# Two pairs' first-half block of scores in the other half of the array's columns, with a second copy of v's first 64 rows

## The reference

```python
# B, H, S, D = 2, 8, 768, 48: r, k, v, w are [B, H, S, D], u is [H, D]
for t in range(S):
    cur = u * k[t] (outer) v[t]
    y[t] = r[t] . (state + cur)
    state = w[t] * state + k[t] (outer) v[t]
x = y as [1536, 384]
x = elu(x @ w_in) @ w_out                        # 384 -> 2048 -> 384
out = sum_e p[:, e] * (relu(x @ w1[e]) @ w2[e])  # 4 experts, 384 -> 1024 -> 384
```

## Time and profile before

| | |
|---|---|
| median of 3 runs | 646.93 us (646.88 to 647.08) |
| the profiled execution | 646.69 us, its span 644.9 us |
| PE busy | 638.4 us of the span (99%) |
| DVE busy | 418.6 us (65%) |
| ACT busy | 237.1 us (37%) |
| POOL busy | 296.0 us (46%) |

### The profile page before, as it was taken

How to read it: one execution, slowest core, us unless ns; L and a number is a source line. 1 busy time by engine, 2 the same in 40 slices (tenths; PEclk the granted TensorE clock), 3 DMA queues, 4 the chain that set the end, 5 groups by cost and what they waited for, 6 DMA issues and landing times.

```text
span 644.9 us, 13796 instructions
## 1 busy us (share of the span) xinstructions
PE 638.4 (99%) x5046; PEld 591.5 (92%) x5046; DVE 418.6 (65%) x786; ACT 237.1 (37%) x557; POOL 296.0 (46%) x370
## 2 busy tenths in 40 slices
PE   8999999999999999999999999999999999999998
PEld 5998999877788888999999999999999999999997
DVE  7889999865357666565655555565656565656564
ACT  4785555655455554222222222222222222222221
POOL 5897424420499999996029900029900018000000
PEclk9999999999999999999999999999999999999999
DMA  8954454300000233000012100013100011001011
GB/s 322 403 193 137 138 183 164 124 11 1 1 2 1 73 98 99 27 1 1 1 50 99 50 1 0 1 49 99 50 1 0 0 50 50 0 1 49 0 50 50
DMA packets 19043, 42.34 MB, mean 66 GB/s; under 512 B 2608, under 2 KB 8752, under 8 KB 18992
## 3 DMA queue, kind: packets, MB, share of 16 engines
q1 hardware_dynamic: 18704, 41.23, 18.6%
q10 hardware_dynamic: 288, 0.39, 0.2%
HBM read 37.16 MB, written 4.46 MB: 65 GB/s over the span
## 4 chain that ended last, share of the span: by engine, by line
PE 90%; DVE 4%; POOL 3%; issue 1%; DMA 0%; ACT 0%; DVEq 0%; POOLq 0%
PE bank L1365 29%; PE bank L1366 29%; PE bank L1367 29%; POOL w_lo L546 3%; PE bank L1199 1%; PE bank L1278 1%; DVE fr L863 1%; PE bank L1290 1%; DVE fr L882 1%; DVE att L921 0%; DMA rkw<-rkw_dram 0%; DVE w_lo L966 0%; DVE bank L996 0%; PE bank L1232 0%; PE bank L1298 0%
## 5 line engine op out<-in xcount | busy, mean ns | idle before, releaser
L1365 PE MATMUL bank<-x_lo,w_hi 128*128 128x256 f32 (+2 forms) x416 | 138.1, 332 | 0.5 <-POOL w_lo L546 0.3
L1366 PE MATMUL bank<-x_hi,w_lo 128*128 128x256 f32 (+2 forms) x416 | 135.2, 325 | 0.0
L1367 PE MATMUL bank<-x_hi,w_hi 128*128 128x256 f32 (+2 forms) x416 | 135.2, 325 | 0.0
L1366 PE MATMUL bank<-w_hi,g_lo 128*128 128x384 f32 x384 | 129.6, 338 | 0.0
L1367 PE MATMUL bank<-w_hi,g_hi 128*128 128x384 f32 x384 | 129.3, 337 | 0.0
L1365 PE MATMUL bank<-w_lo,g_hi 128*128 128x384 f32 x384 | 129.0, 336 | 0.0
L826 ACT ACTIVATE g_hi<-bank 128x512 fp32r<-128x512 f32 x96 | 57.5, 598 | 144.3 <-DVE bank L1052 122.4
L1365 PEld LDWEIGHTS bank<-x_lo,w_hi 128*128 128x128 f32 x416 | 78.2, 188 | 10.4 <-issue 2.5
L1367 PEld LDWEIGHTS bank<-x_hi,w_hi 128*128 128x128 f32 x416 | 78.3, 188 | 7.4
L1366 PEld LDWEIGHTS bank<-x_hi,w_lo 128*128 128x128 f32 x416 | 78.3, 188 | 7.1
L1045 DVE TENSOR_TENSOR u_sum<-p_copy,bank 128x256 f32<-128x256 f32 x56 | 23.6, 421 | 92.1 <-ACT p_copy L750 91.3
(11 more groups left out here) (134 smaller groups left out, 1258.8 us busy)
## 6 DMA issues: line engine op xcount, KB each, us to landing
raw<-w_dram SPq DMA_DIRECT2D x48, 384.0 KB, 3.7
rkw<-rkw_dram SPq DMA_DIRECT2D x10, 772.5 KB, 4.5
tok<-tok_dram SPq DMA_DIRECT2D x10, 576.0 KB, 5.9
k_blocks_dram<-k_blocks SPq DMA_DIRECT2D x8, 256.0 KB, 4.1
kt_sb<-k_blocks_dram SPq DMA_DIRECT2D x32, 64.0 KB, 2.0
out_dram<-acc SPq DMA_DIRECT2D x10, 192.0 KB, 1.9
rkw<-rkw_dram SPq DMA_DIRECT2D x2, 512.0 KB, 4.4
rkw<-rkw_dram SPq DMA_DIRECT2D x2, 260.5 KB, 3.3
```

The source lines that it names most:

```text
L1365: pe.matmul(out, wh, ml, start=start, stop=False, skip_group_check=shared)
L1366: pe.matmul(out, wl, mh, start=False, stop=False, skip_group_check=shared)
L1367: return pe.matmul(out, wh, mh, start=False, stop=stop, skip_group_check=shared)
```

## The change

For chunks 2 to 11, and in each of them for the pairs 0 and 1 (the "exchanged" pairs), the block of first-half keys by first-half queries is computed in the second half of the array's columns, so that it comes out in PSUM partitions 64 to 127, where the fully masked block lay. The fully masked block isn't computed for any pair. All blocks but one for each of the pairs 2 and 3 have now 64 queries. An exchanged pair's strips then take two matmuls of 64 queries instead of one of 128: for the first-half queries with a stationary operand whose rows 64 to 127 hold v's first 64 rows (`twice`, loaded by SP as two copies into `bonus_v_sb`), for the others with v as before. `copy_odd` copies the odd part of `twice` too. The pairs stand in another order in the score banks and in `att` (`place`), and the mask is a pair of masks, side by side; the exchanged one is put together by three more transfers. The reduction behind the diagonal writes its sums in that order.

```diff
+            def load_twice(c):
+                sp.wait_ge(s_py, c - 1)
+                sp.wait_ge(s_odd, odd_done(c - 2))
+                early = tok_d[c][0:HALF, 2 * DM:2 * DM + DM // 2]
+                sp.dma_start(twice(c), early.unsqueeze(0).broadcast_to([2, HALF, DM // 2])).then_inc(s_twice[c % 2], 16)
...
-            sp.dma_start(const[:, :], const_d).then_inc(s_const, 16)
+            sp.dma_start(const[:, P:3 * P], const_d[:, C_MASK:C_MASK + 2 * P]).then_inc(s_const, 16)
...
             load_slices(10, 11, 12, 13, 14, 15)
+            earlier, later = slice(0, HALF), slice(HALF, CH)
+            sp.dma_start(const[:, later], const_d[:, later]).then_inc(s_exchanged, 16)
+            sp.dma_start(const[earlier, earlier], const_d[later, earlier]).then_inc(s_exchanged, 16)
+            sp.dma_start(const[later, earlier], const_d[earlier, earlier]).then_inc(s_exchanged, 16)
+            load_twice(FIRST)
             sp.dma_start(probs[:, :, :], probs_d).then_inc(s_probs, 16)
             for c in range(4, NC):
                 load_rkw(c)
                 load_tok(c)
+                load_twice(c - 1)
                 move_blocks(c - 2)
+            load_twice(NC - 1)
...
+                if c >= FIRST:
+                    twice_landed(act, c)
+                    odd = twice(c).rearrange("p (a e) -> p a e", e=PD)[:, :, D:D + STRIP // 2]
+                    act.copy(v_odd[:, c % 2, PAIRS:, STRIP // 2:STRIP], odd).then_inc(s_odd, 1)
...
-                    dve.copy_predicated(att[:, o, :, :], masks.bitcast(I32), found).then_inc(s_att, 1)
+                    found = banks["x"][o][:, :].rearrange("p (a t) -> p a t", a=PAIRS // 2)
+                    dve.copy_predicated(att[:, o, :, :].rearrange("p (a b) t -> p a (b t)", b=2),
+                                        both_masks.unsqueeze(1).broadcast_to([P, PAIRS // 2, 2 * CH]).bitcast(I32),
+                                        found).then_inc(s_att, 1)
...
-                        for half in range(2):
-                            keys = slice(p * CH + HALF * half, p * CH + HALF * half + HALF)
-                            ins = pe.matmul(banks["x"][o][HALF * half:HALF * half + HALF, cols], k[rows, keys],
-                                            q[rows, cols], start=True, stop=True)
+                def block(p, o, at, keys, first, count):
+                    rows, out = slice(64 * o, 64 * o + D), place(c, p) * CH + first
+                    return pe.matmul(banks["x"][o][HALF * at:HALF * at + HALF, out:out + count],
+                                     k[rows, p * CH + HALF * keys:p * CH + HALF * keys + HALF],
+                                     q[rows, p * CH + first:p * CH + first + count], start=True, stop=True)
+                for p in range(PAIRS // 2):
+                    whole, apart = p + PAIRS // 2, p
+                    for o in range(2):
+                        block(whole, o, 0, 0, 0, CH)
+                    for o in range(2):
+                        block(whole, o, 1, 1, HALF, HALF)
+                    for o in range(2):
+                        block(apart, o, 1, 1, HALF, HALF)
+                    for o in range(2):
+                        block(apart, o, 0, 0, HALF, HALF)
+                    for o in range(2):
+                        ins = block(apart, o, 1, 0, 0, HALF)
...
+            def strip(c, yt, o, b, columns, v, v_twice):
+                to = strip_of(yt, b)[0:columns]
+                found = att[:, o, place(c, b // 3), :]
+                if exchanged(c, b // 3):
+                    pe.matmul(to[:, 0:HALF], v_twice, found[:, 0:HALF], start=False, stop=True, skip_group_check=True)
+                    return pe.matmul(to[:, HALF:CH], v, found[:, HALF:CH], start=False, stop=True, skip_group_check=True)
+                return pe.matmul(to, v, found, start=False, stop=True, skip_group_check=True)
```

More of the change, by code:

```diff
@@ L223, in bass_linear_attention_elu_ffn_dense_experts @@
         s_const = sem("s_const")
+        s_exchanged = sem("s_exchanged")
+        s_twice = [sem(f"s_twice{i}") for i in range(2)]
         s_probs = sem("s_probs")
@@ L294, in bass_linear_attention_elu_ffn_dense_experts, with twice, twice_landed, odd_done @@
         s_dr = sem("s_dr")
-        mask = const[:, C_MASK:C_MASK + P]
-        ident = const[:, C_ID:C_ID + P]
+        both_masks = const[:, 0:2 * P]
+        mask = const[:, P:2 * P]
+        ident = const[:, 2 * P:3 * P]
         def landed(eng, sems, c):
             eng.wait_ge(sems[c % DEEP], 16 * (c // DEEP + 1))
+        def twice(c):
+            return bonus_v_sb[:, c % 2, 0:DM // 2]
+        def twice_landed(eng, c):
+            eng.wait_ge(s_twice[c % 2], 16 * (c // 2 - FIRST // 2 + 1))
+        def odd_done(c):
+            return c + 1 + max(c + 1 - FIRST, 0)
+        def exchanged(c, p):
+            return c >= FIRST and p < PAIRS // 2
+        def place(c, p):
+            return p if c < FIRST else p % 2 * 2 + p // 2
         def raw_q(c):
@@ L1189, in scores @@
                 q, k = q_of(c), k_of(c)
-                for p in range(PAIRS):
-                    cols = slice(p * CH, (p + 1) * CH)
-                    for o in range(2):
[L1193 to L1196, removed]
-                        for half in range(2):
-                            keys = slice(p * CH + HALF * half, p * CH + HALF * half + HALF)
-                            ins = pe.matmul(banks["x"][o][HALF * half:HALF * half + HALF, cols], k[rows, keys],
-                                            q[rows, cols], start=True, stop=True)
+                if c < FIRST:
+                    for p in range(PAIRS):
+                        cols = slice(p * CH, (p + 1) * CH)
+                        for o in range(2):
+                            rows = slice(64 * o, 64 * o + D)
+                            ins = pe.matmul(banks["x"][o][:, cols], k[rows, cols], q[rows, cols], start=True, stop=True)
+                    ins.then_inc(s_px, 1)
+                    return
+                def block(p, o, at, keys, first, count):
[5 more added lines that the diff above has]
+                    whole, apart = p + PAIRS // 2, p
+                    for o in range(2):
+                        block(whole, o, 0, 0, 0, CH)
[7 more added lines that the diff above has]
+                        ins = block(apart, o, 1, 0, 0, HALF)
                 ins.then_inc(s_px, 1)
@@ L1282, in values_even, with twice_part @@
+            def twice_part(c, b, part):
+                return twice(c)[:, part] if exchanged(c, b // 3) else None
             def values_even(c, yt):
                 landed(pe, s_tok, c)
+                if c >= FIRST:
+                    twice_landed(pe, c)
                 pe.wait_ge(s_att, c * 2 + 1)
-                v = v_of(c)
                 for b in (0, 1, 6, 3, 4, 9, 10, 7):
-                    p, first = b // 3, b * STRIP
                     columns = STRIP // 2 if b % 3 == 1 else STRIP
-                    pe.matmul(strip_of(yt, b)[0:columns], v[:, first:first + columns], att[:, 0, p, :],
-                              start=False, stop=True, skip_group_check=True)
+                    part = slice(b * STRIP, b * STRIP + columns)
+                    strip(c, yt, 0, b, columns, v_of(c)[:, part], twice_part(c, b, part))
@@ L1293, in odd_strip @@
             def odd_strip(c, yt, b):
-                return pe.matmul(strip_of(yt, b), v_of(c)[:, b * STRIP:(b + 1) * STRIP], att[:, 1, b // 3, :],
-                                 start=False, stop=True, skip_group_check=True)
+                part = slice(b * STRIP, (b + 1) * STRIP)
+                return strip(c, yt, 1, b, STRIP, v_of(c)[:, part], twice_part(c, b, part))
             def odd_end(c, yt, b):
-                return pe.matmul(strip_of(yt, b), v_odd[:, c % 2, b // 3, :], att[:, 1, b // 3, :],
-                                 start=False, stop=True, skip_group_check=True)
+                return strip(c, yt, 1, b, STRIP, v_odd[:, c % 2, b // 3, :], v_odd[:, c % 2, PAIRS + b // 3 % 2, :])
```

25 lines of the change are left out of this document (14 added, 11 removed).

## The result

The changed kernel takes 650.28 us (median of 6 runs, 649.31 to 650.87), the one before in the same session 646.90 us (6 runs, 646.73 to 647.08): ratio 1.005, 95% interval 1.0039 to 1.0060. I had 646.0, and 645.2 to 647.2 as the range. The profiled execution took 650.52 us with a span of 648.7, 3.8 us more than the span before.

What follows compares the result with a forecast made beforehand. PE, busy 99% of the span, was taken as the bound, except where POOL or DVE holds it. From 646.93 us, 1.12 spared less 0.16 added and about 0.05 waited gave 646.0 us, range 645.2 to 647.2.

Steps and rivals of the forecast that it cites:

- The transfer that isn't quite hidden: SP's loop: 96 KB ahead of the k blocks' write, 0.24 us at 400 GB/s; `update` waits 0.05 to 0.1 us.
- the second: Rival, chance 0.17: slower masks, or `kt_sb` late by another 0.3 us in chunks 5 to 7, take the gain back.
- Chunk 2's slack: Queue behind the weights: mask transfers and chunk 2's `twice` land by 34.5 us, first used at 39.96, hidden by 5 us.
- The scores: PE's score blocks, chunks 5 to 11 counting: 0.16 us spared a chunk, between 0.11 and 0.21; 64-query rounds of 0.059 us.
- The strips: PE's split strips, eight chunks counting: 0.02 us added a chunk, if the column groups work on independently.
- the rival of 652.8: Rival, chance 0.05: split strips run one after another, up to 0.11 us each, 0.88 us a chunk, giving 652.8 us.
- the strict order: PE's matmuls: the Trainium skill's rule of a strict queue without reordering, by which successive strips to one group wait.
- Masks, copy, DVE: DVE's masks and reduction keep their times; ACT's second copy, below 0.23 us, is hidden beside 1.35 us of masks.
- the DVE-bound stretch: 44.7 to 68.8 us, chunks 3 and 4: DVE busy 22.6 of 24.1 us, so a faster PE only waits longer.
- The sum: Whole kernel: 1.12 us spared in scores, 0.16 added in strips, about 0.05 waited, so 0.9 us gained.

Runs made afterwards that it cites:

- e3: The kernel before with the changed kernel's single `twice` transfers added, which nothing reads: 651.07 us, ratio 1.0086.
- e6: e5 with the two matmuls of each split strip issued apart, first ones of four strips, then second ones: 646.57 us, ratio 0.9995.
- e9: e6 with 24 early matmuls of 2 columns that do no useful work, to move instruction fetches: 646.87 us, ratio 0.9996.
- e11: e5 with 24 early matmuls of 2 columns that do no useful work, to move instruction fetches: 647.44 us, ratio 1.0005.
- e12: e6 with 12 idle fp32 matmuls of 2 columns (48 instructions) just ahead of chunk 2's scores: 646.01 us, ratio 0.9987.
- e5: e1 with the k blocks' write and reads issued ahead of the loads of `tok` and `twice` in SP's loop: 647.10 us, ratio 1.0002.
- e7: e5 with no strip split, so some queries get the wrong rows of v: 647.10 us, ratio 1.0006.
- e1: The changed kernel with each `twice` sent as two transfers of 64 rows instead of one: 647.67 us, ratio 1.0011.
- e2: The changed kernel with the single `twice` transfer issued behind the k blocks' write and reads: 648.28 us, ratio 1.0019.
- e4: The kernel before with the `twice` transfers added as two of 64 rows each, read by nothing: 647.16 us, ratio 1.0005.
- e8: The kernel before with `load_tok` moved behind the k blocks' write and reads in SP's loop: 646.92 us, ratio 1.0000.

## Why the prediction was wrong, point by point

- **The step that failed** is "The transfer that isn't quite hidden", and in it the line "0.24 us at 400 GB/s" for the 96 KB ahead of the write. It priced the transfer by its bytes over all engines. It went through two of them, at 51 GB/s, and held the write behind it: 2.0 us more in chunk 6 (6.6 against 4.5), and in all 4.4 us of waits where I had 0.05 to 0.1 (chunk 6's 1.1 us of them needed a fetch of instructions as well). e3 shows it alone. A transfer through few engines wasn't among the rivals; the second had the right place ("`kt_sb` late by another 0.3 in chunks 5 to 7") and about a quarter of the size in each chunk. The diff showed the cause: the source is read as `[2, 64, 192]`, and the two copies are its outermost dimension. The Trainium skill (DMA: Bandwidth & Descriptors, Rules for kernel authors) states it for this very form: "a leading zero-stride broadcast of c copies" confines a DMA "to at most c engines". The trace agrees, with two signals of landing, 51 GB/s, and the write's last two signals 1.6 us behind its other 14. I had not weighed that rule.
- **Chunk 2's slack** of 5 us was taken for the mask and `twice` themselves. They were hidden; the write of chunk 2's k blocks in the same queue was not. That write is the 9.24 us in the chain, and 2.2 of the 4.4 us: what I asked was when the new data are needed, not what is queued behind them.
- **The scores** were right: 0.176 us spared a chunk for 0.16, within 0.11 to 0.21 (12 rounds of 0.064 make 0.77, so the lower end should read 0.10). Rounds of 64 take 58 ns, for 59.
- **The strips** were mis-sized: 0.083 us for 0.02 (and 0.025 in `update`, for nothing). The column groups do work on independently, as the earlier trace rows show. The changed kernel shows it too: in chunk 6 L1353 starts at 94.24, ahead of L1352's records at 94.33, which stand before it in the code. So the rival of 652.8 and the strict order that is quoted beside it fell, by 0.083 us measured against 0.88; e6 has 0.015, the 0.02 of the sum. The rest is the order in which the matmuls are issued, which the sum left out.
- **Masks, copy, DVE** were right: the mask's median goes from 731 to 742 ns, the second copy takes 213 ns, and PE's delay shrinks in the DVE-bound stretch from 2.33 to 1.9 us (chunk 4's old values), as spare time of PE lies there.
- **Fetches** were in no step. By e9, e11 and e12 they are the wait of 0.3 to 1.1 us in chunk 4 of e5, e6 and e7, and most of what e5 and e7 missed their expected times by. The ones in chunk 6 of the changed kernel, e1 and e2 were read from the times alone.
- **The sum** holds when its errors are mended: e12 is 0.9 us under the kernel before, in the runs' medians and 0.73 in PE's place at chunk 11. That is the 0.9 that I had forecast for the change, but in part by luck: e12 spares 0.016 us a chunk more in the scores than the sum has, loses 0.2 us in chunk 2 and 0.1 in chunk 8, which it hasn't, and has another order on SP and on PE, two transfers for one, and 48 idle instructions.

What stays open: that a fetch and the read or write beside it used the same DMA engine is read from their times, not shown; whether the fetches that fall within the long writes of chunks 2 and 5 (at 40.3 and 77.5 us) lengthened them isn't known; chunk 2's 0.2 us behind `w_lo` wasn't traced to its cause, and as it is in e3, e4 and e8 too, where PE does what it did before, it isn't the new blocks'; and the stop beside an early fetch was seen in two profiles only (0.83 us in e9, 0.6 in e11), without a cause.

## What to carry to other kernels

Price a new transfer by the engines it will run on: look at the outermost dimension of both sides, keep the 128 or 64 rows there, and split a copy made twice into two transfers. Then ask what is queued behind it, not only when its own data are needed: here the victim was another transfer. When a unit works in groups side by side, issue the first piece of every group before the second of any, and when a wait appears far from an edit in a kernel with no slack, look at where the instruction fetches have moved.

## What the hardware showed that I had not expected

- A transfer of 128 packets of 768 bytes on two DMA engines takes 2.5 us; as two transfers of 64 rows its packets pass in 1.8 us beside another load.
- A fetch of 16 KB of instructions is one DMA packet of 0.9 to 1.9 us. A 256 KB write of 2.0 us took 0.5 to 1.6 us longer when one came just behind its issue, and a read of 2.0 us took 1.3 to 1.5 us longer in chunk 6 of three kernels.
- With 48 matmuls of 2 columns at 8 us the clock went to its lower level for some 10 us in the profile, and the mean clock was 0.989 to 0.995 in four runs of six; with 24 it stayed at 1.00 in the profile.
- Of a write that shares two of its 16 engines with a slow transfer, 14 signals came by 89.95 us and the last two at 91.56 and 91.59.
